# Six sets of tile buffers, one scatter a tile, and four late tiles placed by float32r products

## What is computed

```python
# attention with decay: B=2, H=8, S=768, D=48
for t in range(S):
    cur = einsum('bhd,bhe->bhde', u[None] * kt, vt)
    y[:, :, t] = einsum('bhd,bhde->bhe', rt, state + cur)
    state = w[None, :, :, None] * state + einsum('bhd,bhe->bhde', kt, vt)
# x = y as 1536 tokens of 384; 8 experts, capacity 384
logits = x @ w_gate
expert_idx = argmax(logits, axis=1)
for i in range(N):                      # token i gets the next free slot of its expert
    e = expert_idx[i]
    if counts[e] < capacity:
        disp[e, counts[e]] = x[i]; pos[i] = counts[e]; counts[e] += 1; keep[i] = True
h = maximum(einsum('ecd,edf->ecf', disp, w1), 0.0)
y = einsum('ecf,efd->ecd', h, w2)
out[i] = gate_w[i] * y[expert_idx[i], pos[i]]     # 0 where not kept
# then, over all tokens: h = x @ w_in; solu = h * softmax(h); layer norm * g_ln; @ w_out
```

## Time and profile before

| | us |
|---|---|
| median of 3 runs | 335.09 (333.76 to 336.6) |
| the profiled execution | 335.23, of which the span is 333.5 |
| from the span's start to tile 11's key-query products | 72.68 |
| from there to the first expert product | 12.34 |
| experts and last stage, from the first expert product | 248.5 (333.5 - 85.02) |

### The profile page before, as it was taken

One profiled execution on the slowest core, in us unless ns is written; L12 is line 12 of the kernel. 1 busy time (PEld: TensorE's weight loads), 2 busy tenths in 40 slices (PEclk: granted clock), 3 DMA queues, 4 the chain that ended last, 5 costly groups with the idle time before them and its releaser, 6 DMA issues.

```text
span 333.5 us, 7114 instructions
## 1 busy us (share of the span) xinstructions
PE 310.2 (93%) x2660; PEld 279.4 (84%) x2662; DVE 212.7 (64%) x471; ACT 196.4 (59%) x374; POOL 187.0 (56%) x168
## 2 busy tenths in 40 slices
PE   7697978988999999999999999799999999999991
PEld 4486767867999999999999999688999999999991
DVE  7764763789855656464554556889897666656610
ACT  2485774878585766766676757256556445533520
POOL 4865677872698988989898969400031111111131
PEclk9999997999999999999999999989999999999998
DMA  8999999994397939494766685000000000000010
GB/s 136 155 261 245 251 226 182 279 398 154 115 372 264 337 130 342 127 300 176 242 197 225 212 266 187 1 0 1 2 25 26 24 24 26 24 26 24 25 44 33
DMA packets 62901, 50.70 MB, mean 152 GB/s; under 512 B 42512, under 2 KB 58256, under 8 KB 62864
## 3 DMA queue, kind: packets, MB, share of 16 engines
q1 hardware_dynamic: 59104, 45.25, 47.2%
q0 software_dynamic: 1920, 4.73, 3.9%
q10 hardware_dynamic: 1840, 0.21, 0.8%
HBM read 38.37 MB, written 11.82 MB: 150 GB/s over the span
## 4 chain that ended last, share of the span: by engine, by line
PE 78%; issue 8%; POOL 7%; DVE 3%; ACT 1%; DMA 1%; POOLq 0%; SPq 0%; DVEq 0%
PE ps L1372 25%; PE ps L1648 15%; PE ps L1665 15%; PE ps L1373 12%; PE ps L1674 3%; POOL own_place L568 2%; PE ps L1445 2%; POOL own_place L575 2%; POOL place L583 1%; PE ps L1366 1%; PE ps L1494 1%; PE ps L1505 1%; POOL place L611 1%; DMA wsq<-in_w_dram 1%; PE ps L1570 1%
## 5 line engine op out<-in xcount | busy, mean ns | idle before, releaser
L511 POOL TENSOR_TENSOR w_lo<-w_raw,w_hi 128x768 fp32r<-128x768 f32 x33 | 60.5, 1859 | 10.3 <-DVE w_lo L517 9.8
L1372 PE MATMUL ps<-xe,w_hi 128*128 128x448 f32 x192 | 61.9, 378 | 0.3
L1372 PE MATMUL ps<-h,w_hi 128*128 128x448 f32 x192 | 61.8, 378 | 0.0
L1665 PE MATMUL ps<-w_hi,h 128*128 128x384 f32 x192 | 51.5, 340 | 0.0
L1373 PE MATMUL ps<-h,w_lo 128*128 128x224 f32 x192 | 50.7, 264 | 0.0
L1373 PE MATMUL ps<-xe,w_lo 128*128 128x224 f32 x192 | 50.7, 264 | 0.0
L1648 PE MATMUL ps<-w_hi,xe 128*128 128x512 f32 x144 | 47.7, 402 | 2.0 <-DVE xe L1219 2.0
L672 POOL TENSOR_TENSOR rstd<-var_b,minus_half 128x1 f32<-128x1 f32 x12 | 6.8, 565 | 74.6 <-DVE var_b L1318 74.6
L954 DVE TENSOR_TENSOR ps<-ps,rk_in 128x448 f32<-128x448 f32 x32 | 20.2, 632 | 32.9 <-ACT rk_in L726 32.9
L1372 PEld LDWEIGHTS ps<-xe,w_hi 128*128 128x128 f32 x192 | 36.0, 188 | 5.0 <-issue 2.0
L517 POOL TENSOR_TENSOR w_lo<-w_raw,w_hi 128x1024 fp32r<-128x1024 f32 x16 | 38.2, 2411 | 1.9 <-DVE w_lo L517 1.9
(11 more groups left out here) (165 smaller groups left out, 612.3 us busy)
## 6 DMA issues: line engine op xcount, KB each, us to landing
w_raw<-in_moe_w_dram SPq DMA_DIRECT2D x15, 1536.0 KB, 7.8
x_slots<-zeros SPq DMA_DIRECT2D x6, 768.0 KB, 6.0
rk_in<-in_r_dram SPq DMA_DIRECT2D x12, 192.0 KB, 5.3
rk_in<-in_k_dram SPq DMA_DIRECT2D x12, 192.0 KB, 5.9
v_in<-in_v_dram SPq DMA_DIRECT2D x12, 192.0 KB, 5.2
out_dram<-zeros SPq DMA_DIRECT2D x1, 2304.0 KB, 8.1
w_raw<-in_moe_w_dram SPq DMA_DIRECT2D x3, 512.0 KB, 5.3
rows_in<-x_slots SPq DMA_DIRECT2D x8, 192.0 KB, 8.0
```

Of the source, the lines that this page charges most:

```text
L511: eng.tensor_tensor(w1_lo[:, :, cols], w1_raw[:, i, :, cols], w1_hi[:, :, cols].bitcast(F32), ALU.subtract).then_inc(g.w1_lo, 1)
L1372: pe.matmul(ps[:, bank, 0:2 * n], w_hi, x[:, c, 0:2 * n], start=first, stop=False, skip_group_check=True)
L1665: last = pe.matmul(ps[:, OB + i, 0:DM], ht[:, f, i * P:(i + 1) * P], wt[:, f, :], start=(f == 0 and z == 0), stop=(f == KF - 1 and z == 2))
```

## The change

1. NB is 6. Four sets stay in rk_in and v_in, two more (more_in) lie in the second set of w1_raw, reached by rk_of and v_of. Their pads are cleared by one more memset on VectorE, and turn_rk(4) waits for it.
2. load_w1(1, 1), whose place these two sets take, moves behind load_rows(0, 0) and a wait for the last tile's y.
3. GpSimd scatters at most one tile a round, up to tile 10's round.
4. LATE is four tiles, 8 to 11, and GROUPS is 0-2, 3-5, 6-7, 8, 9, 10, 11.
5. A late tile's x is rounded to float32r by ScalarE (late_hi), GpSimd makes the remainder, and place_late multiplies both with columns_of: six float32r products a tile for three float32 ones. late_x and columns_of lie in h.
6. The loaded rows are transposed ahead of the last tile's place_late, which now closes the banks and releases them.
7. VectorE takes decay_r(t + 1) ahead of add_own(t + 1).

```diff
-    NB = 4
+    NB = 6
+    IN_PLACE = 4
...
-        LATE = [NT - 3, NT - 2, NT - 1]
-        columns_of = scores[:, 0].rearrange("p a h t -> p (a h t)")[:, 0:3 * N1].rearrange("p (t n) -> p t n", t=3)
+        LATE = [NT - 4, NT - 3, NT - 2, NT - 1]
+        h_place = h[:].rearrange("p f n -> p (f n)")
+        late_x = h_place[:, 0:2 * len(LATE) * DM].rearrange("p (t z d) -> p t z d", t=len(LATE), z=2)
...
+        more_in = w1_raw[:, 1].rearrange("p c f -> p (c f)")[:, 0:(NB - IN_PLACE) * 3 * H * DP]\
...
+        def rk_of(i):
+            return rk_in[:, i] if i < IN_PLACE else more_in[:, i - IN_PLACE, 0:2]
...
-        GROUPS = [range(0, 3), range(3, 6), range(6, 9), range(9, 10), range(10, 11), range(11, 12)]
+        GROUPS = [range(0, 3), range(3, 6), range(6, 8), range(8, 9), range(9, 10), range(10, 11), range(11, 12)]
...
             for a in range(1, ZERO_PARTS):
                 zero_slots(a)
-                load_tile(NB - 1 + a)
-            for t in range(NB - 1 + ZERO_PARTS, NT):
+                load_tile(NB + a - 1)
+            for t in range(NB + ZERO_PARTS - 1, NT):
                 load_tile(t)
             for a in range(KD):
                 load_first_w1(a)
             load_w2(0, 0)
-            load_w1(1, 1)
...
             sp.wait_ge(scattered, 16 * LATE[0])
             load_rows(0, 0)
+            sp.wait_ge(y_done, NT)
+            load_w1(1, 1)
...
-                for _ in range(2):
-                    if t >= GROUPS[group_of(stored)][-1] + 4:
-                        if stored == 0:
-                            pool.wait_ge(slots_zeroed, 16 * ZERO_PARTS)
-                        scatter(stored)
-                        stored += 1
+                if t < NT - 1 and t >= GROUPS[group_of(stored)][-1] + 4:
+                    if stored == 0:
+                        pool.wait_ge(slots_zeroed, 16 * ZERO_PARTS)
+                    scatter(stored)
+                    stored += 1
             for t in range(stored, LATE[0]):
                 scatter(t)
+            for j in range(len(LATE)):
+                pool.wait_ge(late_x_hi, j + 1)
+                pool.tensor_tensor(late_x[:, j, 1], x_rows(LATE[j]), late_x[:, j, 0].bitcast(F32), ALU.subtract)\
+                    .then_inc(late_x_lo, 1)
...
+            def late_hi(j):
+                act.wait_ge(x_ready, LATE[j] + 1)
+                act.activation(late_x[:, j, 0], x_rows(LATE[j]), ACT.Copy).then_inc(late_x_hi, 1)
...
+                    late_hi(0)
+                    late_hi(1)
                     act_w1_hi(act, 0, usual.w1_in[0], w1_loads(0, 1), usual.w1_hi, parts=[0])
                     take_x(t - 1)
...
             put_first_diagonal()
+            dve.memset(more_in.rearrange("p a b h d -> p (a b h) d")[:, :, D:DP], 0.0).then_inc(more_pads_ready, 1)
...
                 if 0 < t < NT - 1:
+                    decay_r(t + 1)
                     add_own(t + 1)
-                    decay_r(t + 1)
...
                 pe.wait_ge(columns_ready, j + 1)
-                pe.wait_ge(x_ready, LATE[j] + 1)
+                pe.wait_ge(late_x_lo, j + 1)
                 for c in range(KD):
-                    pe.matmul(first_turned(c), x_rows(LATE[j])[:, c * P:(c + 1) * P], columns_of[:, j],
-                              start=(j == 0), stop=False, skip_group_check=True)
+                    for z in range(2):
+                        last = pe.matmul(first_turned(c), late_x[:, j, z, c * P:(c + 1) * P], columns_of[:, j],
+                                         start=(j == 0 and z == 0), stop=(j == len(LATE) - 1 and z == 1), skip_group_check=True)
+                    if j == len(LATE) - 1:
+                        last.then_inc(usual.xe_turned, 1)
...
             place_late(0)
+            place_late(1)
             count_before(len(GROUPS) - 1)
-            place_late(1)
             place_late(2)
             place_first_rows()
+            place_late(3)
```

More of the change, by code:

```diff
@@ L71, in decay_attention_moe_solu @@
         zeros = sb("zeros", [P, DM])
-        rk_in = sb("rk_in", [P, NB, 2, H, DP])
-        v_in = sb("v_in", [P, NB, H, DP])
+        rk_in = sb("rk_in", [P, IN_PLACE, 2, H, DP])
+        v_in = sb("v_in", [P, IN_PLACE, H, DP])
         place = sb("place", [P, KD * YW])
@@ L142, in decay_attention_moe_solu, with v_of @@
         h = sb("h", [P, KF, 4 * P], F32R)
-        LATE = [NT - 3, NT - 2, NT - 1]
-        columns_of = scores[:, 0].rearrange("p a h t -> p (a h t)")[:, 0:3 * N1].rearrange("p (t n) -> p t n", t=3)
+        LATE = [NT - 4, NT - 3, NT - 2, NT - 1]
+        h_place = h[:].rearrange("p f n -> p (f n)")
+        late_x = h_place[:, 0:2 * len(LATE) * DM].rearrange("p (t z d) -> p t z d", t=len(LATE), z=2)
+        columns_of = h_place[:, 2 * len(LATE) * DM:2 * len(LATE) * DM + len(LATE) * N1].rearrange("p (t n) -> p t n", t=len(LATE))
         column_key = rows_in[:, 1].rearrange("p m d -> p (m d)")[:, 0:N1]
         column_key_i = rows_in[:, 0].rearrange("p m d -> p (m d)")[:, 0:N1].bitcast(I32)
+        more_in = w1_raw[:, 1].rearrange("p c f -> p (c f)")[:, 0:(NB - IN_PLACE) * 3 * H * DP]\
+            .rearrange("p (a b h d) -> p a b h d", a=NB - IN_PLACE, b=3, h=H)
+        def rk_of(i):
+            return rk_in[:, i] if i < IN_PLACE else more_in[:, i - IN_PLACE, 0:2]
+        def v_of(i):
+            return v_in[:, i] if i < IN_PLACE else more_in[:, i - IN_PLACE, 2]
         def x_rows(t):
@@ L304, in decay_attention_moe_solu @@
         columns_ready = sem("columns_ready")
+        late_x_hi = sem("late_x_hi")
+        late_x_lo = sem("late_x_lo")
         late_rank = sem("late_rank")
@@ L817, in _ @@
             gate_exp(len(GROUPS) - 2)
+            late_hi(2)
             act_w1_hi(act, 0, usual.w1_in[0], w1_loads(0, 1), usual.w1_hi, parts=[1])
             take_x(NT - 1)
+            late_hi(3)
             act_w1_hi(act, 0, usual.w1_in[0], w1_loads(0, 1), usual.w1_hi, parts=[2, 3])
@@ L1172, in _ @@
                         add_picked(n)
-            late_columns(0)
-            rank_late(1)
+                        if g[-1] == LATE[0]:
+                            late_columns(0)
+            late_columns(1)
+            rank_late(2)
             add_picked(len(GROUPS) - 2)
@@ L1178, in _ @@
             pick_experts(len(GROUPS) - 1)
-            late_columns(1)
-            rank_late(2)
             late_columns(2)
+            rank_late(3)
+            late_columns(3)
             late_slots()
@@ L1451, in turn_rk @@
                 pe.wait_ge(loaded[i], 32 * (t // NB + 1))
+                if t == IN_PLACE:
+                    pe.wait_ge(more_pads_ready, 1)
                 if t > 0:
                     pe.wait_ge(r_decayed, t)
-                turn(RT, rk_in[:, i, 0]).then_inc(r_turned, 1)
+                turn(RT, rk_of(i)[:, 0]).then_inc(r_turned, 1)
                 if t == 0:
-                    turn(KT, rk_in[:, i, 1]).then_inc(k_turned, 1)
+                    turn(KT, rk_of(i)[:, 1]).then_inc(k_turned, 1)
                 else:
@@ L1494, in state_update @@
                     last = pe.matmul(ps[part, UB, DP * (h // 2):DP * (h // 2 + 1)], k_last[:, t % 2, h, :],
-                                     v_in[:, t % NB, h, :], start=True, stop=True)
+                                     v_of(t % NB)[:, h, :], start=True, stop=True)
                 last.then_inc(update_done, 1)
@@ L1513, in own_keys_out @@
                 for h in range(H) if t < NT - 1 else EVEN_PAIRS + ODD_PAIRS:
-                    last = pe.matmul(y_place(h), v_in[:, t % NB, h, :],
+                    last = pe.matmul(y_place(h), v_of(t % NB)[:, h, :],
                                      scores[:, t % 2, h % 2, h // 2, :], start=(c == 0 and h < 4), stop=(h >= H - 4),
@@ L1578, in place_first_rows @@
                     for m, rows in enumerate(usual.rows):
-                        last = pe.matmul(first_turned(c)[:, m * P:m * P + rows], rows_in[0:rows, 0, m, c * P:(c + 1) * P],
-                                         ident[0:rows, 0:rows], start=False, stop=(m == 1), skip_group_check=True)
-                    last.then_inc(usual.xe_turned, 1)
+                        pe.matmul(first_turned(c)[:, m * P:m * P + rows], rows_in[0:rows, 0, m, c * P:(c + 1) * P],
+                                  ident[0:rows, 0:rows], start=False, stop=False, skip_group_check=True)
             pe.wait_ge(zero_ready, 1)
```

12 lines of the change are left out of this document (6 added, 6 removed).

## The result

The changed kernel takes 342.7 us (median of 4 runs, 340.16 to 343.09); the kernel before, measured beside it, 335.85 (333.76 to 338.5). The ratio is 1.0184 with a 95% interval of [1.0093, 1.0275]: slower. All ratios here are worked out over the fast runs of both kernels and are not the quotients of the two medians (1.0204 here). Its profiled execution took 343.09 us with a span of 341.2, against 335.23 and 333.5 before.

What follows compares the result with a forecast made beforehand. TensorE was taken to bound the kernel, with its idle time in the attention stage. The terms 5.4 - 0.2 + 0.5 gave +5.7 us on the median of 335.09, so 340.8 us, with a range of 337.0 to 344.0.

Steps and rivals of the forecast that it cites:

- The main step: Tile 7's round: zeroing, behind two more tiles, ends at 54.2; GpSimd's first scatter waits 10.8 us; T(8) +5.4 us.
- The price of 6.1 to 6.9 us for two tiles: SyncE's queue: two more tiles (1.18 MB) at 172 to 193 GB/s delay the last zeroing store; 6.7 us taken.
- rival 2: Zeroing queue: two tiles cost only 3.2 us, zeroing in at 50.7, kernel 337.3 us, no measurable change; chance 0.12.
- Rival 1: Zeroing stores run beside the tile loads, T(8) at 49.6, kernel faster at 327.9 us; chance 0.10.
- The term for the clock: Tile 7's round, after TensorE's long idling: restarting at the 1.2 GHz level adds 0.1 us before T(8).
- Rounds 8 to 10: Attention rounds with one scatter each: 4.7 + 5.2 + 5.5 = 15.4 us against 15.6, so -0.2 us.
- rival 3: GpSimd becomes the bound in tiles 8 to 10's rounds, adding 1.5 to 3 us: 342.5 to 344; chance 0.15.
- The tail: From tile 11's key-query products to the first expert product: +0.5 us, between -0.6 and +1.5.
- GpSimd's four subtractions: Between T(11) and the first expert: 1.0 us each, hidden in GpSimd's 5.95 us wait for the rows.
- the cheaper place_late of the other three tiles: Before the first expert: cheaper products, but ahead of the rows' landing, so worth nothing.
- rival 4: Before the first expert: another step late, second expert's w1 by over 3 us or the rows; over 344; chance 0.05.
- the forecast proper: Whole kernel: the prediction's main case, between 338.2 and 342.5 us, given chance 0.58.

Runs made afterwards that it cites:

- e2: The kernel before, four sets of buffers kept, with only SyncE's order of tiles and zeroing from the changed kernel: 339.87 us, ratio 1.0277 to before.
- e1: The changed kernel with SyncE's order of zeroing stores and tiles put back as in the kernel before: 333.13 us, ratio 1.0065 to before.
- e8: The changed kernel with one tile fewer queued ahead of the last zeroing store: 338.33 us, ratio 1.0178 to before.
- e0: The changed kernel, same code, timed again in a later set of runs: 339.75 us, ratio 1.0298 to before.
- e5: e1 with the late tiles' remainders made by VectorE instead of GpSimd: 332.15 us, ratio 1.0000 to before.
- e10: e5 with seven unused products by zeros added on TensorE in the tail: 330.82 us, ratio 0.9963 to before.
- e4: The changed kernel with GpSimd's first scatter behind own_parts(9) instead of own_parts(7): 332.13 us, ratio 1.0011 to before.
- e6: e4 with the late tiles' remainders made by VectorE instead of GpSimd: 330.07 us, ratio 0.9938 to before.
- e9: e6 with seven unused products by zeros added on TensorE in the tail: 328.71 us, ratio 0.9892 to before.
- e3: The changed kernel with 44 unused products by zeros filling TensorE's idle time in tile 7's round: 339.6 us, ratio 1.0279 to before.

## Why the prediction was right, and where its sizes were not

**The main step was right.** The zeroing was to end at 54.2 and ended at 54.83, GpSimd was to wait 10.8 us and waited 10.92, and no key wait in round 3 was left. e2 shows that this step alone makes the loss, e1 that taking it out gives back 6.6 us of 8.5, e8 that it rises with the number of tiles. The price of 6.1 to 6.9 us for two tiles was that of the earlier trace rows, where besides 0.32 MB of loads 0.04 MB of a scatter were in flight; the last store was issued 7.9 us later and landed 7.4 later. By the ceiling of 435 GB/s of the Trainium skill ("DMA: Bandwidth & Descriptors", section "Specifications") it would, as an estimate, have been in at about 50.2. The traces do not agree: e0's 50.94 comes near, but the landing without the two tiles varies too (45.77 in e1, 45.60 in e5, 44.85 in e10), and from e1 to e0, timed side by side, the two tiles cost 5.2 us, and 3.5 between the nearest pair (47.47 and 50.94), where the ceiling gives 2.7. That the landing of one kernel varies by 4 us was in no step of mine; one trace can't show it. So the close hit of 54.2 is in part luck: in e0 the release came before 51, my sign for rival 2, and the kernel still was 8.5 us slower.

**Rival 1** (zeroing beside the loads) fell: the store waited in the queue. Without the wait T(8) is at 52.0, 51.3 and 51.1 (e4, e6, e9), not at its 49.6, so even then it would have been some 2 us too good.

**The term for the clock was mis-sized.** "I add 0.1 us" to the 5.43 us between the state's part of y and T(8); measured 6.41. T(8) came at 64.15, outside the 61.5 to 63.5 given as a sign; of the 1.65 us over 62.5, 0.6 are the later landing and 0.9 this. The step took the low clock of before as if it were the whole of it. But 5.43 already held a mixture (0.50 at 52 to 53, 0.82 at 55 to 56 in the earlier trace rows), and after a stop of ten microseconds nearly all of it ran at 1.2 GHz. e3 gives the other end, 3.93: so before had paid some 1.5 us and the changed kernel 2.5.

**Rounds 8 to 10 had the wrong sign.** "-0.2" was +0.3 (15.91; 15.82 in e0, 15.84 in e1; 15.61 in e2, with the scatters of before). One scatter a round, with the rest of the change in those rounds, costs a little, and rival 3 (1.5 to 3 us) did not come.

**The tail was the wrong term.** "+0.5, between -0.6 and +1.5" was +2.9 (after) to +3.8 (e1). Two steps failed in it. First, GpSimd's four subtractions were to cost nothing in its wait of 5.95 us for the rows: GpSimd had the time, but they held up VectorE, a neighbour I did not look at (2.02 us for 0.23 in e0). Second, the cheaper place_late of the other three tiles was booked as worth nothing: TensorE, less busy, lost its clock in the stretch that follows, in all traces with the changed tail but the first and the two with seven more products. That the cheaper products are the reason is argued and not tested. e5 takes out the first, worth 0.65% of the time, and e10 the lower clock, worth about 0.4%. The sign of over 13.5 us from T(11) that I had tied to rival 4 did appear, with neither w1 nor the rows late; only in e9, with all else repaired, did the rows end last. In the execution of *after* itself the tail's clock was 1.00 and its 2.9 us went otherwise (VectorE's masking of tile 11 waited 2.48 us, which no other trace repeats), so its split is not that of e0; what held tile 11 up there stays open.

**The total was nearer than the steps deserved, and that is luck.** The total of +10.3 us at the first expert product is well over the +5.7 forecast. The whole span was only 7.7 us longer (341.2 against 333.5), because before's profiled execution, against which the sum was made, was itself 2.6 us long behind that point. The 342.7 lies over the 338.2 to 342.5 of the forecast proper, in the band of rival 3, which did not come. And e0, beside its own runs of before, puts the loss at 8.5 us; on the 335.09 of the forecast that would be 343.6, and its ratio 1.0298 would give 345.1, over the upper end of the range.

**The version that beats both** is e9, 1.1% faster than before: six sets for the tiles, the scatters held back until the zeroing is in, the remainders on VectorE, and seven products by zeros. e6, without the seven, is 0.6% faster.

## What to carry to other kernels

When loads are moved ahead in a queue, look for who waits for what now stands behind them, and what stands behind that waiter; moving the waiter (e4, 1.0011) was here at least as good as moving the transfer (e1, 1.0065). Put no GpSimd arithmetic beside short vector instructions on the critical path, however idle GpSimd is. And when cheaper products leave TensorE partly idle, read the granted clock of the stretch that follows before booking the gain.
